# Factor loads and the first two units of the last stage, taken apart: a change at two seams of a float32 attention and MoE chain

## The reference

```python
def _attn_ref(q, k, v, g_norm):                 # q, k, v: 8 batches, 8 heads, 576 tokens, 64
    kv = np.einsum('bhsd,bhse->bhde', k, v)
    out = np.einsum('bhsd,bhde->bhse', q, kv)
    rms = np.sqrt(np.mean(out * out, axis=-1, keepdims=True) + 1e-06)
    return (out / rms * g_norm)

def _moe_ref(x, w_gate, w_val, w_out):          # x: 4608 tokens x 512; hidden 1536
    gate = 1.0 / (1.0 + np.exp(-(x @ w_gate)))
    val = x @ w_val
    return (gate * val @ w_out)

def _moe2_ref(x, w_in, w_out):                  # hidden 2048
    h = x @ w_in
    g = np.where(h >= 1, h, np.where(h <= -1, 0.0, (h + 1) ** 2 / 4))
    return (g @ w_out)

# out = moe2(moe(attention(q, k, v)))
```

## Time and profile before

| | |
|---|---|
| median of 3 runs | 1707.41 us (1705.03 to 1708.48) |
| the profiled execution | 1706.1 us, its span 1704.3 us |
| mean granted TensorE clock | 0.991 of full speed |
| TensorE busy with matmuls | 1658.4 us, 97% |
| VectorE, ScalarE, GpSimd busy | 1216.3, 886.0, 202.2 us |
| moved in DRAM | 156.76 MB read, 120.06 MB written |

### The profile page before, as it was taken

One profiled execution on the slowest core, in us unless ns is written; L12 is line 12 of the kernel. 1 busy time (PEld: TensorE's weight loads), 2 busy tenths in 40 slices (PEclk: granted clock), 3 DMA queues, 4 the chain that ended last, 5 costly groups with the idle time before them and its releaser, 6 DMA issues. The chain is left out here.

```text
span 1704.3 us, 31798 instructions
## 1 busy us (share of the span) xinstructions
PE 1658.4 (97%) x12475; PEld 1627.3 (95%) x12475; DVE 1216.3 (71%) x1725; ACT 886.0 (52%) x1612; POOL 202.2 (12%) x266
## 2 busy tenths in 40 slices
PE   8999999999999999999999999999997899999999
PEld 6789999999999998999999999999997799999999
DVE  3677777777777775877778787777775577777664
ACT  4666666655555554544445555555553444444442
POOL 3410000015242221200002500000002100000000
PEclk9999999999999999999999999999998999999999
DMA  7444444334777777744334333333439844444451
GB/s 256 153 136 140 146 140 140 111 128 133 245 242 239 240 264 238 242 154 153 116 136 164 133 133 132 140 121 122 162 134 318 276 124 125 143 138 140 124 124 38
DMA packets 229317, 278.91 MB, mean 164 GB/s; under 512 B 33072, under 2 KB 172848, under 8 KB 229168
## 3 DMA queue, kind: packets, MB, share of 16 engines
q1 hardware_dynamic: 217104, 233.35, 41.4%
q0 software_dynamic: 12064, 43.52, 7.8%
HBM read 156.76 MB, written 120.06 MB: 162 GB/s over the span
## 5 line engine op out<-in xcount | busy, mean ns | idle before, releaser
L1542 PE MATMUL x<-t_hi,v_lo 128*128 128x288 f32 x1664 | 498.6, 300 | 19.0 <-ACT c_kept L1009 11.5
L1543 PE MATMUL x<-t_lo,v_hi 128*128 128x288 f32 x1664 | 493.7, 297 | 0.0
L1544 PE MATMUL x<-t_hi,v_hi 128*128 128x288 f32 x1664 | 492.3, 296 | 0.0
L1542 PEld LDWEIGHTS x<-t_hi,v_lo 128*128 128x128 f32 x1664 | 314.2, 189 | 24.3 <-ACT c_kept L1009 12.2
L1544 PEld LDWEIGHTS x<-t_hi,v_hi 128*128 128x128 f32 x1664 | 315.3, 190 | 0.0
L1543 PEld LDWEIGHTS x<-t_lo,v_hi 128*128 128x128 f32 x1664 | 314.5, 189 | 0.1
L1542 PE MATMUL y<-t_hi,v_lo 128*128 128x288 f32 x832 | 250.2, 301 | 5.7 <-DVE c L1087 1.7
L1543 PE MATMUL y<-t_lo,v_hi 128*128 128x288 f32 x832 | 247.0, 297 | 0.0
L1544 PE MATMUL y<-t_hi,v_hi 128*128 128x288 f32 x832 | 246.5, 296 | 0.0
L1542 PE MATMUL x<-v_hi,t_lo 128*128 128x256 f32 x576 | 164.0, 285 | 5.2 <-DMA v_lo<-fold_lo 2.8
L1542 PEld LDWEIGHTS y<-t_hi,v_lo 128*128 128x128 f32 x832 | 157.5, 189 | 10.4 <-DVE c_tile L1087 3.7
(11 more groups left out here) (187 smaller groups left out, 3520.8 us busy)
## 6 DMA issues: line engine op xcount, KB each, us to landing
g_scratch<-c_tile SPq DMA_DIRECT2D x128, 288.0 KB, 2.4
gq<-g_scratch SPq DMA_DIRECT2D x64, 512.0 KB, 6.1
h_scratch<-gate SPq DMA_DIRECT2D x192, 144.0 KB, 1.8
hq<-h_scratch SPq DMA_DIRECT2D x32, 864.0 KB, 5.1
stage<-w_in POOLq DMA_DIRECT2D x68, 256.0 KB, 3.3
kv_ring<-kv_in SPq DMA_DIRECT2D x30, 512.0 KB, 4.5
fold_hi<-fold_hi SPq DMA_DIRECT2D x14, 896.0 KB, 6.0
fold_lo<-stage SPq DMA_DIRECT2D x14, 896.0 KB, 4.9
```

Source lines behind the costliest of these rows:

```text
L1542: nc.tensor.matmul(dst, s_lo, m_hi, start=start, stop=False, skip_group_check=True)
L1543: nc.tensor.matmul(dst, s_hi, m_lo, start=False, stop=False, skip_group_check=True)
L1544: return nc.tensor.matmul(dst, s_hi, m_hi, start=False, stop=stop, skip_group_check=True)
```

## The change

Three edits. First, a fold task is split like every other: its hi and lo parts go to seven chunks of the ring which are free in the second half of A (28 to 34 for even tasks, 35 to 41 for odd ones), and are stored from there. ScalarE's cast then waits for the stores of the task two before; GpSimd's loads into `stage` wait only for the split. `load_b(0)` and `load_b(1)` move behind task 26's sums. SP's wait for the stores of h at step 88 comes before step 87's stores and covers the steps before it.

Second, `load_d`: the first six half factors go one per step; x = 6 and 7 wait for the arrival of unit 1's last quarter but one in the queue (`gq_loaded[1][3]`), and from x = 8 each half waits for a product of unit 0 (two halves for each).

Third, units 0 and 1 of stage D run product by product in turns (`SEQ`): (unit 0, first product), (unit 1, first product), (unit 0, second), and so on, so that a factor serves two products in a row. Their buffers are laid out anew (`c_tile` as three single tiles in another order, `gq[1]`, a second `s_sum` and a second set of `o_kept`), each quarter has a semaphore of its own, quarters 0 and 2 of unit 1 are loaded in the last block of C, quarters 3 and 1 at its end, and unit 2's quarters one by one. From unit 2 on the order is as before.

```diff
+SEQ = [(u, i) for i in range(SEVEN) for u in range(2)] + [(u, i) for u in range(2, UNITS) for i in range(SEVEN)]
+AT = {item: e for e, item in enumerate(SEQ)}
+D_SUMS = [(0, 1), (0, 4), (0, 2), (1, 1), (1, 4), (1, 2), (0, 5), (1, 5)] + [
+    (u, i) for u in range(2, UNITS) for i in (1, 4, 2, 5)]
...
+    if task < C_TASK:
+        return parts(28 + SEVEN * (task % 2), SEVEN)
...
-                sp.dma_start(fold_place(task, 0), fold_hi[:].bitcast(f32)).then_inc(fold_stored[task % 2], 16)
+                sp.dma_start(fold_place(task, 0), fold_chunks(v_hi, task)).then_inc(fold_stored[task % 2], 16)
...
+                if k == A_STEPS - 8:
+                    all_stored(sp, h0_stored, k - 1, 16)
+                    all_stored(sp, h1_stored, k - 1, 16)
                 if k:
                     store_h0(k - 1)
...
                 if k == A_STEPS - 8:
-                    all_stored(sp, h0_stored, k, 16)
-                    all_stored(sp, h1_stored, k, 16)
                     load_quarter_h(0)
                 elif k == A_STEPS - 6:
-                    for i in range(2):
-                        sp.wait_ge(fold_stored[i], 32 * (C_TASK - FOLD1_TASK) // 2)
                     load_quarter_h(3)
...
                     elif b == C_BLOCKS - 1 and s in (2, 5):
-                        load_quarter(1, (2, 3)[s // 3])
+                        load_quarter(1, (0, 2)[s // 3])
+                    if b == C_BLOCKS - 1 and s == C_SETS - 1:
+                        sp.wait_ge(g_stored[1], 32 * len(range(1, C_STEPS, 3)))
+                        load_quarter(1, 3)
                     store_hidden(C_SETS * b + s)
-            for x in range(2):
-                i = (C_STEPS - 3 + x) % 3
-                sp.wait_ge(g_stored[i], 32 * len(range(i, C_STEPS, 3)))
-                load_quarter(1, x)
...
+            sp.wait_ge(g_stored[2], 32 * len(range(2, C_STEPS, 3)))
+            load_quarter(1, 1)
+            for x, last in ((0, (1, 2)), (1, (0, 3)), (2, (0, 4)), (3, (0, 6))):
+                sp.wait_ge(s_ready, AT[last] + 1)
+                load_quarter(2, x)
...
             def load_d(x):
-                pool.wait_ge(p_done[3], D0 - C_SETS + (4 * x + 3) // SEVEN + 1)
-                if x >= 10:
-                    pool.wait_ge(p_done[1 if x < 12 else 5], D0 + 1)
+                if x < 6:
+                    pool.wait_ge(p_done[3], D0 - C_SETS + x + 1)
+                elif x < 8:
+                    pool.wait_ge(gq_loaded[1][3], 16)
+                else:
+                    pool.wait_ge(p_done[ORDER_D[x // 2 - 3]], D0 + 1)
+                    if x >= 12:
+                        pool.wait_ge(p_done[3], D0)
...
             def split_weights(task):
                 act.wait_ge(stage_summed, 4 * (task + 1))
-                if is_fold(task):
-                    if task == FOLD1_TASK:
-                        act.wait_ge(x_ready, 8 * B)
-                    for earlier in range(max(FOLD1_TASK, task - 2), task):
-                        act.wait_ge(fold_stored[earlier % 2], 32 * len(range(FOLD1_TASK + earlier % 2, earlier + 1, 2)))
-                    nc.scalar.copy(fold_hi[:], stage[:, task % 2, :, :]).then_inc(v_hi_done, 1)
-                    return
...
+                elif FOLD1_TASK <= task < C_TASK:
+                    act.wait_ge(fold_stored[task % 2], 32 * ((task - FOLD1_TASK) // 2))
...
-                    split_d_item(0, 1)
-                    sum_d_item(0, 5)
+                    split_d_item(1)
+            split_d_item(2)
             finish(C_STEPS - 1)
-            split_d_item(0, 4)
+            sum_d_item(1, 1)
+            split_d_item(3)
+            split_d_item(4)
+            sum_d_item(1, 4)
+            sum_d_item(1, 2)
+            sum_d_item(0, 5)
...
-            for u in range(UNITS):
-                g = D0 + u
-                pe.wait_ge(c21_ready, g - 1 - B0)
-                d_product(u, 1, X, True)
...
+            for u, j in SEQ:
+                number, g = ORDER_D[j], D0 + u
+                if number == 1:
+                    pe.wait_ge(c21_ready, g - 1 - B0)
+                    d_product(u, 1, X, True)
...
```

More of the change, by code:

```diff
@@ L252, in program @@
         g_stored = [sem(f"g_stored{i}") for i in range(3)]
-        gq_loaded = [sem(f"gq_loaded{i}") for i in range(2)]
+        gq_loaded = [[sem(f"gq_loaded{i}{x}") for x in range(4)] for i in range(2)]
         s_summed = sem("s_summed")
@@ L1049, in _, with keep @@
                     nc.scalar.activation(c_sq[:], c_sq[:], ACT.Square, bias=half_col[:, 0:1], scale=0.5).then_inc(square_ready, 1)
-            split_d_item(4)
-            def keep(slot, u, source, done, freed, kept_now):
+            for e in range(3, D_SLOTS):
+                split_d_item(e)
+            def keep(slot, u, source, done, kept_now):
                 act.wait_ge(done, D0 + u + 1)
-                act.wait_ge(freed, D0 + u)
-                nc.scalar.copy(o_kept[:, slot, :], source[u % 2][:, 0:R]).then_inc(kept_now, 1)
@@ new lines, in keep @@
+                nc.scalar.copy(o_kept[u % 2][slot][:], source[u % 2][:, 0:R]).then_inc(kept_now, 1)
+            for p, (u, j) in enumerate(SEQ):
+                number = ORDER_D[j]
+                if number == 1:
+                    if u == 0:
+                        for ready in (c11_ready, c12_ready, c22_ready):
+                            act.wait_ge(ready, D0)
+                    elif u > 1:
+                        act.wait_ge(c22_ready, D0 + u - 1)
+                    keep(0, u, X, p_done[1], p1_kept)
+                elif number == 5:
+                    keep(1, u, Y, p_done[5], p5_kept)
+                elif number == 6:
+                    if u > 1:
+                        act.wait_ge(c12_ready, D0 + u - 1)
+                    keep(2, u, X, p_done[6], u2_kept)
+                elif number == 7:
+                    act.wait_ge(c11_ready, D0 + u + 1)
+                    keep(0, u, X, p_done[7], u3_kept)
+                elif number == 4:
+                    act.wait_ge(p_done[4], D0 + u + 1)
+                    if u == 0:
+                        act.wait_ge(g_ready, C_STEPS)
+                        act.wait_ge(g_stored[0], 32 * len(range(0, C_STEPS, 3)))
+                    reach(act, out_stored[u % 2], 32 * (u // 2))
+                    nc.scalar.copy(o_tile[u % 2][:, 1, 0:R], X[u % 2][:, 0:R]).then_inc(c21_ready, 1)
+                if p + D_SLOTS < len(SEQ):
+                    split_d_item(p + D_SLOTS)
@@ L1093, in split_weights @@
                 dve.wait_ge(v_hi_done, task + 1)
-                if is_fold(task):
-                    raw = stage[:, task % 2, :, :]
-                    low(raw.bitcast(f32r), raw, fold_hi[:]).then_inc(v_ready, 1)
-                    return
                 for base, first, count in chunk_pieces(task):
@@ new lines, in _ @@
+            sum_d_item(1, 1)
[4 more added lines that the diff above has]
+            sum_d_item(0, 5)
+            for p, (u, j) in enumerate(SEQ):
+                number = ORDER_D[j]
+                o = o_tile[u % 2]
+                first, kept5, kept2 = (part[:] for part in o_kept[u % 2])
+                if number == 2:
+                    dve.wait_ge(p_done[2], D0 + u + 1)
+                    dve.wait_ge(p1_kept, D0 + u + 1)
+                    if u == 0:
+                        dve.wait_ge(g_ready, C_STEPS)
+                        dve.wait_ge(g_stored[0], 32 * len(range(0, C_STEPS, 3)))
+                    reach(dve, out_stored[u % 2], 32 * (u // 2))
+                    add(o[:, 0, 0:R], Z2[u % 2][:, 0:R], first).then_inc(c11_ready, 1)
+                elif number == 7:
+                    dve.wait_ge(p5_kept, u + 1)
+                    dve.wait_ge(u3_kept, D0 + u + 1)
+                    add(o[:, 1, R:], kept5, first).then_inc(c22_ready, 1)
+                elif number == 3:
+                    dve.wait_ge(p_done[3], D0 + u + 1)
+                    dve.wait_ge(u2_kept, D0 + u + 1)
+                    add(o[:, 0, R:], Y[u % 2][:, 0:R], kept2).then_inc(c12_ready, 1)
+                if p + D_SLOTS < len(SEQ):
+                    nu, i = SEQ[p + D_SLOTS]
+                    if nu > 1:
+                        for item in ((1, 4), (2,), (5,), (), (), (), ())[i]:
+                            sum_d_item(nu, item)
+                    elif (nu, i) == (1, 3):
+                        sum_d_item(1, 5)
+                    split_d_item(p + D_SLOTS)
```

226 lines of the change are left out of this document (92 added, 134 removed).

## The result

The changed kernel takes 1683.28 us (median of 5 runs, 1679.3 to 1686.53), the kernel before, timed beside it, 1705.42 us (5 runs, 1704.2 to 1708.48). The ratio is 0.9867, 95% interval 0.9851 to 0.9884: 22 us or 1.3% faster. Forecast were 1681 us and a range of 1676 to 1691. The profiled execution took 1682.83 us, its span is 1681.0.

The account below looks back on a forecast made before the run. TensorE, busy 1658.4 of 1704.3 us, was taken as the bound, so edits win its waits and slow clock. Terms 4.7 + 3.4 + 10.8 + 2.6 + 3.2 = 24.7 us off 1706.1 gave 1681 us, range 1676 to 1691.

Parts of the forecast that it names:

- fold tasks by way of the ring: Stage A, window 450 to 500: the cast's wait for the previous task's stores goes, 4.7 of 5.4 us won.
- end of stage A: Window 637 to 651: later factor loads and SP's moved wait let stores land before VectorE needs them, 3.4 us won.
- one half factor per step: Stage C's tail: fewer bytes per step remove the 9.3 us wait and the slow stretch behind it, 10.8 us won.
- end of stage C: Block 2-2: VectorE's sum moves behind the stage, TensorE's wait shrinks and the clock should not fall, 2.6 us won.
- beginning of stage D: Units 0 and 1 in turns, each factor serving two products: 3.0 us lost instead of 6.2, 3.2 won.
- the wait ahead of step 87's stores: End of stage A: added wait for step 86's stores, with step 87's stores and a load VectorE needs queued behind it.
- T + 39: Stage D, 39 us after its first product's start (T): unit 2's quarters, slowed beside factor loads, have all landed.
- item 3's: Stage D, unit 1's second item: due at T + 8.6, ready at T + 9.6, 1.0 us late.
- item 7's: Stage D: due at T + 20.2, about 1.3 us late because `gq11` lands late and VectorE must first make a sum.
- Starved quarters: Rival, start of stage D: small-packet quarters beside eight half factors lose half as much again as before; 1687 us, chance 0.14.
- Stage A gives nothing: Rival, stage A: stores land late for another reason and other waits follow; 1689 us, chance 0.09.
- nothing: Rival, seam of stages C and D: bound by bytes, so the gains vanish and a wait comes on top; 1706, chance 0.04.

Follow-up runs that it names:

- no late factors: Changed kernel without GpSimd's loads of the last six half factors (x = 8 to 13), output not the reference's: 1678.46 us in one run.
- Both orders: Changed kernel, VectorE making item 14's low part before unit 2's sums and ScalarE copying `o_tile` before casting items 15 and 16: 1677.13 us, again 1678.47.
- pace alone: Kernel before, with only the first eight half factors of stage C released one per step: 1699.43 us against 1705.78, ratio 0.9956.

## Why the prediction held, and where it did not

The sum was right within the spread of the runs (1681 forecast, 1683.3 measured), and not each of its terms. In the first profile luck helps: 2.9 us in places that no edit touches nearly make up for the term that failed. Forecast and measured, in the two profiles of the changed kernel, and once more against the mean of the profiles with the old code:

| term | forecast | ledger | against the mean |
|---|---|---|---|
| fold tasks by way of the ring | 4.7 (3 to 5.4) | 4.0, 4.7 | 4.2, 4.9 |
| end of stage A | 3.4 (0 to 3.7) | 3.9, 3.9 (1.9 to 4.2 in seven others with the same stage A) | 3.4, 3.4 |
| one half factor per step | 10.8 (3 to 10.8) | 10.7, 10.7 | 11.9, 11.9 |
| end of stage C | 2.6 (1.2 to 2.9) | 2.0, 2.0 | 1.6, 1.7 |
| beginning of stage D | 3.2 | -0.2, -0.3 | 1.5, 1.4 |
| places not touched | 0 | 2.9, 0.5 | |

- **The fold tasks** went as said: the casts of the window follow a 0.45 us instruction without a wait, and one wait of 1.1 us on `gate`, at step 59, is left.
- **The end of stage A** came out in size, and both of its reasons are needed, but they are one: I wrote them side by side, and neither gives anything without the other. What I had taken for a risk, the wait ahead of step 87's stores, comes together with the load of h leaving earlier. Code that is the same gave 1.9 to 4.2 us here, so the term is not better known than that.
- **The pace** gave its upper end, and the stores of the tail landed in 3.9 us as the sum of bytes per step had it. What the prediction lacked is that a part of this gain, of a size that stays open, depends on stage D's new order.
- **The end of stage C** gave somewhat less than forecast, though its clock stayed up (1.00); only the wait of 0.5 us on the copy `c_kept` is left in TensorE's list.
- **The beginning of stage D** is the term that failed. The step is "Unit 2's quarters crawl beside them and are all there near T + 39; its first item is due at T + 40 plus what was lost: 0.5 to 1 us more." The landing was right: T + 39.3. But the sentence counted the way from the quarter to unit 2's first *item*, and not what else stands behind the wait on the two in-order engines. That was 4.16 us of waiting and a slow stretch behind it, the sign that the prediction had named as wrong ("a wait of over 3 us at unit 2's first item"). From T to unit 2's third copy it is 56.7 us, and 50.3 in "no late factors", 0.7 of which is its wait at item 3: the changed kernel loses 7.1 us there, and I had 3.0. Both orders turned round, the D seam gives 4.4 and 5.9 us, which is more than the 3.2 of the forecast. Of the smaller waits, item 3's was forecast at 1.0 us and measured at 0.7 and 1.1; item 7's, forecast at 1.3, did not occur.
- **Rivals.** "Starved quarters" (1687) came nearest: D lost 7.1 us, where it had half as much again as the 6.2 counted before. Starvation made one quarter late, and the order behind it made that cost 4 us and a slow clock; take away either, and most of the loss is gone. "Stage A gives nothing" and "nothing" are out by the ledger's columns. Of "nothing" one part lives on: with pace alone, a part of what the stall had cost comes back in stage D.

## What to carry to other kernels

When a transfer is forecast to be late, list everything that is queued behind the first instruction that waits for it, on each in-order engine, and above all the short copies that free a bank or a buffer; put those and all work that needs nothing of the transfer ahead of it. Where two edits share a queue, price them together and test each alone: here one part made the kernel 0.12% faster, the other 0.04% slower, neither clear of no change, and both together 0.4% faster. And look at the due times behind a release pace: pacing loads to save the stage before can cost the next stage, unless it needs them later. Last, take more than one profile of the kernel before: here code that was the same differed by 3.4 us in the very stretch of which the forecast was 3.2.

## What the runs showed of the hardware

- The same wait can cost the clock or not. At the seam of stages A and B 1.87 us pass between the starts of two matmuls in each kernel, 1.6 of them idle, the kernel before among them; in 8 of the 14 profiles the granted clock then fell to its lower level and 1.3 to 1.5 us more were lost, in 6 it did not fall. In "TensorE: Matmul & The Clock Gate" (Part 1) the Trainium skill says that the point at which sustained matmuls bring the higher clock varies from run to run; of a fall behind a short wait, which is what varies here, that passage does not speak. One cannot book such a gain from a single profile.
- Two queues that share the engines move packet for packet, whatever the packets weigh: 804 against 807 in 8 us, 2.62 MB against 0.41. Quarters of 512 KB took a median of 4.3 us without GpSimd's loads and 13.2 beside them, whose packets are larger. Issuing them slows down too: SP was 4.26 and 6.14 us at the issue of single quarters there, and 0.36 without those loads. The longer one, in the changed kernel:

```profile
1336.65 6.14 SPq L548 DMA_DIRECT2D gq<-g_scratch  x1
```

- Why C's steps 0 to 8 vary by 4.6 us in code that nothing here alters is not settled. VectorE waits there for a store of `y_scratch`, and I did not try an edit on it.
